# Two products of the identity with itself ahead of each pair of attention score matmuls

## The chip, the cores and the metric

The kernel runs on one core of one Trainium2 chip. The metric is the device time of one execution in microseconds (us). The kernel before was timed three times: 931.81 us (median), 927.07 us and 935.1 us.

## The reference, cut to what matters

Three stages follow one another: attention with a causal band, a gated feed-forward layer, and four experts that are all applied and weighted.

```python
# attention: q, k, v are (2, 8, 768, 64), n_global 8, n_local 96
scores = scale * np.matmul(q, k.transpose(0, 1, 3, 2))
keep = is_global | is_local            # first 8 keys, or the 96 keys up to the query
scores = np.where(keep, scores + bias, -1e9)       # bias: -slope(head) * distance
a = np.exp(scores - max); a = a / (a.sum + 1e-9)
x = np.matmul(a, v)                    # laid out as (1536, 512)
# feed-forward: w_in (512, 2048), w_out (2048, 512)
h = x @ w_in;  g = h * np.tanh(softplus(h));  x = g @ w_out
# four experts: w1 (4, 512, 1024), w2 (4, 1024, 512), p the normalised shares
out = sum(p[:, e:e + 1] * (np.maximum(x @ w1[e], 0) @ w2[e]) for e in range(4))
```

## The kernel before, in words

It is written engine by engine, with an instruction order laid down by hand and semaphores between the engines. PE is TensorE, DVE VectorE, ACT ScalarE, POOL GpSimd, SP SyncE.

**Attention** takes the 16 heads in 8 pairs of heads (m = 0 to 7). Per pair there are 12 units (u = 0 to 11): six tiles of 128 queries, and for each the two heads, so that units u and u + 1 (u even) are the two heads of one query tile. Since n_local is at most 129 and n_global at most 32, only a band of the keys is worked on: 128 keys for the first query tile, 256 for the second, 288 for the other four (the tile before, the own tile and 32 global keys). A unit goes through these steps:

- **scores** (`scores_of_two`, L517 to L524, matmul at L522): the fp32 product of q and k of both heads of a query tile. Head 0 lies in the rows 0 to 63 of the array, head 1 in the rows 64 to 127. A unit's result goes to PSUM bank u % 3. Before the matmuls, `score_parts` (L490) waits until DVE has read the unit that held the bank before (semaphore `s_ready`).
- **bias and minimum** (`biased`, DVE, L1016), **exp** (`expo`, ACT, L786), **transposes** of the 1 to 3 blocks of 128 keys (`turn`, PE, L538, fp32), the copy out as an fp16 high part (ACT, L810) and low part (DVE, L1131), and the product with v (`pv`, PE, L557, three fp16 matmuls per block).

PE's own order in a pair (`pair`, L561 to L585) is for every u: turn(u); if u is odd, the scores of the two units u + 3 and u + 4 (they reach into the next pair of heads for u = 9 and u = 11); pv of unit u - 1; and after u = 0, 2, 4, 6 a `fill` (L479), which transposes a part of q or k of the next pair. In the last pair `turn_x` (L487) stands in the places of the fills: it transposes the attention's result for the first product. `first` (L526) issues the scores of the units 0 to 3 of the first pair ahead of all. So the scores of an even unit 2, 4, 6, 8 or 10 and its neighbour are issued 40 times in all (1 from `first`, 8 x 4 at u = 1, 3, 5, 7, and 7 at u = 11), and those of unit 0 are issued 8 times.

**Beside attention** the weights are prepared. DVE takes the largest absolute value of w_in and w_out piece by piece (`weights_part`, L970: w_in beside pair 1, w_out beside pair 3). SP spreads each maximum over the partitions with two small DMAs (`share_max`, L407 to L413), behind the loads of q and k in SP's order; DVE makes a scale of it (L1068, L957 to L960; for w_out that is at u = 6 of pair 5), and POOL splits the matrix into fp16 parts with it (L707 to L713). ACT issues the load of w_out at u = 0 of pair 2 (`load_w_out`, L826).

**The rest** (from L587) is the fp16 split products of the feed-forward layer (L597, L620) and of the experts, with their elementwise work on ACT, DVE and POOL. It starts when the last attention output has been scaled (L1056).

Of the kernel before, what the change touches and what calls it, by code (L numbers as in the profile page):

```python
# [13 lines left out]
P = 128  # L14
# [22 lines left out]
def program(nc, q, k, v, n_global, n_local, w_in, w_out, probs, w1, w2, out):  # L37
    B, H, S, D = q.shape
    DM, FF = w_in.shape
    E, _, FE = w1.shape  # L40
# [18 lines left out]
    def offsets(blocks):  # L59
        at, found = 0, []  # L60
        for _, n in blocks:
            found.append(at)
            at += n
        return found, at
# [8 lines left out]
    with ExitStack() as ctx:  # L73
        def sb(name, cols, dt=F32):
            return ctx.enter_context(nc.sbuf_tensor(name, [P, cols], dt))
# [16 lines left out]
        ident = sb("ident", P)  # L92
# [11 lines left out]
        def psum(i, n=GN, at=0):  # L104

            c = 512 * (i % 2) + at
            return bank[i // 2][:, c:c + n]
# [359 lines left out]
        def _(pe):  # L467
# [22 lines left out]
            def score_parts(i, slot, u, banded):  # L490

                blks = (band if banded else full)[u // 2]
                qt, a = u // 2, u % 2
                if u == 0:

                    pe.wait_ge(tr_out, FILLS * (2 * i + slot + 1))
                if banded and (u >= 3 or not isinstance(i, int) or i + slot > 0):
                    pe.wait_ge(s_ready, PB * i + UNITS * slot + u - 2)
                offs, _ = offsets(blks)

                runs = []
                for (kt, n), at in zip(blks, offs):
                    if runs and runs[-1][0] + runs[-1][1] == kt * P and n == P and (at % 512 or not at):
                        runs[-1][1] += P
                    else:
                        runs.append([kt * P, n, at])
                head = slice(a * D, (a + 1) * D)
                return [(psum(u % 3, n, at) if banded else bank[0][:, at:at + n],
                         qT_sb[slot][head, qt * P:(qt + 1) * P], kT_sb[slot][head, key:key + n])
                        for key, n, at in runs]  # L510
# [6 lines left out]
            def scores_of_two(i, slot, u):  # L517

                parts = [score_parts(i, slot, u + a, True) for a in range(2)]
                for n in range(len(parts[0])):  # L520
                    for a in range(2):
                        last = pe.matmul(*parts[a][n], start=True, stop=True)  # L522
                        if n == len(parts[0]) - 1:
                            last.then_inc(s_psum, 1)  # L524

            def first(banded):  # L526
                if banded:
                    scores_of_two(0, 0, 0)
                    scores_of_two(0, 0, 2)
# [31 lines left out]
            def pair(i, slot, banded):  # L561
                for u in range(UNITS):
                    if not banded:
                        scores(i, slot, u, banded)
                    turn(i, slot, u, banded)
                    if banded:
                        ahead, behind = reach(i, slot, u, 3), reach(i, slot, u, -1)
                        if ahead and u % 2:
                            scores_of_two(*ahead)
                        if behind:  # L570
                            pv(*behind, banded)
                    else:
                        pv(i, slot, u, banded)
                    if after(i, slot) and u in FILL_AT:
                        fill(*after(i, slot), FILL_AT.index(u))
                    if not after(i, slot) and u in X0_TURN_AT:
                        c = X0_TURN_AT.index(u)
                        if c == 0:
                            pe.wait_ge(o_ready, 2 + 2 * (PAIRS // 2))
                            pe.wait_ge(tr_out, FILLS * PAIRS)  # L580
                        else:
                            pe.wait_ge(x_ready, c)
                        turn_x(0, c)
                if banded and not after(i, slot):
                    pv(i, slot, UNITS - 1, banded)  # L585
# [781 lines left out]
```

## Time and profile before

| | |
|---|---|
| runs | 931.81 us median (927.07 to 935.1) |
| the profiled execution's own time | 928.6 us |
| its span | 926.8 us |
| mean granted TensorE clock | 0.985 of full speed |
| PE busy | 877.1 us (95% of the span) |
| DVE busy | 524.3 us (57%) |
| ACT busy | 301.4 us (33%) |
| POOL busy | 266.4 us (29%) |
| attention, by PE's timeline | 11 us to 168.6 us |

The span goes from the first to the last instruction; the execution's own time has 1.8 us around it. A granted clock of 1.0 is 2.4 GHz, one of 0.5 is 1.2 GHz. Matmuls are pipelined, and a row's duration of one includes its way through the array, so that several in a row take less than their durations together.

### The profile page before, as it was taken

How to read it: one execution, taken by the hardware profiler on the slowest of the kernel's cores; microseconds unless marked ns; L12 is line 12 of the kernel's file. 1: busy time of each engine (PE TensorE's matmuls, PEld its weight loads, DVE VectorE, ACT ScalarE, POOL GpSimd, SP SyncE). 2: the span in 40 equal slices, each digit the busy share in tenths (PEclk: the TensorE clock that was granted, in tenths of full speed). 3: DMA queues.
4: the chain of work that ended last, by engine and by line, in shares of the span. 5: the costliest groups of instructions: out<-in, count | busy, mean ns of one | idle time of the engine just before them, and what ended most of it. 6: DMA issues, size and time to landing. Idle time of an engine off the chain costs nothing.

```text
span 926.8 us, 12448 instructions
## 1 busy us (share of the span) xinstructions
PE 877.1 (95%) x4880; PEld 441.9 (48%) x4880; DVE 524.3 (57%) x1032; ACT 301.4 (33%) x559; POOL 266.4 (29%) x218
## 2 busy tenths in 40 slices
PE   4887887899999999999999999999999999999998
PEld 3665666544444444444444444444444444444443
DVE  7888866799999999997643214322125322212121
ACT  3565766554455556555020201011010201111020
POOL 1267758022222232231007700049100094000000
PEclk9898989999999999999999999999999999999999
DMA  9735250000000000020100130000400000000001
GB/s 222 233 89 170 66 186 1 1 1 1 1 0 6 4 1 1 4 91 25 70 6 1 57 124 1 6 0 0 181 1 1 6 0 0 0 23 23 34 12 47
DMA packets 52579, 39.30 MB, mean 42 GB/s; under 512 B 41136, under 2 KB 42288, under 8 KB 52016
## 3 DMA queue, kind: packets, MB, share of 16 engines
q1 hardware_dynamic: 50464, 34.44, 12.6%
q10 hardware_dynamic: 2064, 4.19, 1.3%
q8 instruction: 30, 0.49, 0.2%
q14 instruction: 21, 0.17, 0.1%
HBM read 35.48 MB, written 3.15 MB: 42 GB/s over the span
## 4 chain that ended last, share of the span: by engine, by line
PE 66%; DVE 23%; ACT 4%; DMA 4%; issue 2%; POOL 0%; SPq 0%; DVEq 0%; ACTq 0%
PE bank L597 57%; PE bank L620 4%; DVE tmp L1244 4%; DVE tmp L1262 2%; DVE wpieces L970 2%; DVE xT L1260 2%; DVE tmp L1242 2%; DMA wB<-in_moe_w_out 2%; DVE tmp L1248 2%; PE bank L522 2%; PE bank L557 1%; PE bank L538 1%; DVE hid L1254 1%; DVE tmp L1131 1%; ACT tmp L892 1%
## 5 line engine op out<-in xcount | busy, mean ns | idle before, releaser
L597 PE MATMUL bank<-xT,wA 128*128 128x512 f16 (+1 forms) x864 | 194.5, 379 | 1.1 <-DVE acc L1056 1.1
L866 ACT ACTIVATE hid<-bank 128x512 f16<-128x512 f32 x96 | 57.3, 597 | 410.8 <-PE bank L597 410.8
L1235 DVE SCALAR_TENSOR_TENSOR hid<-bank,hid 128x512 f16<-128x512 f32 x96 | 66.4, 691 | 172.5 <-ACT hid L866 172.5
L620 PE MATMUL bank<-hid,wB 128*128 128x512 f16 x576 | 132.1, 379 | 4.3 <-ACT acc L850 2.6
L597 PEld LDWEIGHTS bank<-xT,wA 128*128 128x128 f16 x864 | 84.5, 98 | 102.4 <-DVE acc L1056 1.2
L752 POOL TENSOR_TENSOR tmp<-tmp 128x512 f32<-128x512 f32 x48 | 70.2, 1462 | 196.7 <-DVE tmp L1262 196.7
L597 PE MATMUL bank<-wA,hid 128*128 128x512 f16 x576 | 125.3, 379 | 0.0
L597 PE MATMUL bank<-xT,wB 128*128 x576 | 125.3, 379 | 0.0
L597 PE MATMUL bank<-wB,hid 128*128 128x512 f16 x576 | 125.3, 379 | 0.0
L707 POOL TENSOR_SCALAR stage<-stage,sc 128x1024 f32<-128x1024 f32 x32 | 36.0, 1125 | 251.6 <-DVEq L1228 241.0
L1311 DVE SCALAR_TENSOR_TENSOR acc<-bank,pg,acc 128x512 f32<-128x512 f32 x36 | 27.0, 750 | 131.7 <-PE bank L597 131.7
L620 PEld LDWEIGHTS bank<-hid,wB 128*128 128x128 f16 x576 | 56.1, 98 | 73.0 <-DVE hid L1254 3.5
L597 PEld LDWEIGHTS bank<-xT,wB 128*128 128x128 f16 x576 | 56.4, 98 | 67.9
L597 PEld LDWEIGHTS bank<-wA,hid 128*128 128x128 f16 x576 | 56.4, 98 | 68.0
L597 PEld LDWEIGHTS bank<-wB,hid 128*128 128x128 f16 x576 | 56.3, 98 | 68.0
L886 ACT ACTIVATE hid<-tmp 128x512 f16<-128x512 f32 x48 | 30.3, 630 | 106.5 <-POOL tmp L752 104.6
L597 PE MATMUL bank<-xT,hid 128*128 (+1 forms) x288 | 63.3, 379 | 0.0
L786 ACT ACTIVATE tmp<-tmp 128x288 f32<-128x288 f32 (+2 forms) x96 | 48.5, 505 | 36.2 <-DVE tmp L1016 34.9
L1131 DVE SCALAR_TENSOR_TENSOR tmp<-bank,tmp 128x384 f16<-128x384 f32 (+2 forms) x96 | 46.9, 489 | 23.2 <-ACT tmp L810 23.0
L557 PE MATMUL bank<-xT,tmp 128*128 128x65 f16 x720 | 41.4, 202 | 15.4 <-DVE tmp L1131 14.7
L522 PE MATMUL bank<-hid 64*128 64x256 f32 (+2 forms) x320 | 42.2, 377 | 10.9 <-DVE tmp L1016 10.3
L1244 DVE SCALAR_TENSOR_TENSOR tmp<-tmp 128x512 f32<-128x512 f32 x48 | 48.3, 1007 | 1.6
(105 smaller groups left out, 939.1 us busy)
## 6 DMA issues: line engine op xcount, KB each, us to landing
stage<-in_moe_w SPq DMA_DIRECT2D x8, 2048.0 KB, 10.1
stage<-in_moe_w_in SPq DMA_DIRECT2D x1, 4096.0 KB, 14.3
wB<-in_moe_w_out ACTq DMA_DIRECT2D x1, 4096.0 KB, 18.4
hid<-in_q SPq DMA_DIRECT2D x16, 192.0 KB, 3.5
hid<-in_k SPq DMA_DIRECT2D x16, 192.0 KB, 3.4
xT<-in_v SPq DMA_DIRECT2D x8, 384.0 KB, 4.9
out_y<-acc SPq DMA_DIRECT2D x12, 256.0 KB, 2.0
rows<-max SPq DMA_DIRECT2D x4, 128.0 KB, 4.1
```

The lines of the kernel that those rows point to most:

```text
L522: last = pe.matmul(*parts[a][n], start=True, stop=True)
L557: last = pe.matmul(dst, pt[:, x, b * P:(b + 1) * P], v_parts(m)[:, y, a, kt], start=(b == 0 and n == 0), stop=(b == len(keys) - 1 and n == 2))
L597: last = pe.matmul(dst, lhs(c, a), rhs(c, b), start=(c == 0 and n == 0), stop=(c == chunks - 1 and n == 2))
L620: last = pe.matmul(psum(4 + d), w_out_s[:, a, f // 2, f % 2, d * P:(d + 1) * P], hv[:, T % RING, b, :], start=(f == 0 and n == 0), stop=(f ...
L707: pool.tensor_scalar(tmp, src, scale, 1.0, ALU.mult, ALU.mult).then_inc(w_part, 1)
L752: pool.tensor_tensor(g_t[T % 4], g_t[T % 4], r_t[T % 2], ALU.mult).then_inc(g_ready, 1)
L786: act.activation(t, t, ACT.Exp, bias=nmax[:, u:u + 1], scale=-1.0).then_inc(p_ready, 1)
L866: act.activation(hv[:, f, 0, :], psum(f % 4), ACT.Relu).then_inc(f_hi, 1)
L886: act.activation(hv[:, m % RING, 0, :], g_t[m % 4], ACT.Copy).then_inc(h_hi, 1)
L1131: dve.scalar_tensor_tensor(pt[:, 1], src, P_SCALE, pt[:, 0], ALU.mult, ALU.subtract).then_inc(pT_dve, 1)
L1235: dve.scalar_tensor_tensor(hv[:, f, 1, :], psum(f % 4), 0.0, hv[:, f, 0, :], ALU.max, ALU.subtract).then_inc(f_ready, 1)
L1244: dve.scalar_tensor_tensor(n, u, 2.0, u, ALU.add, ALU.mult).then_inc(n_ready, 1)
```

## The change

In `scores_of_two`, which is called with the first of the two units, u, PE multiplies the fp32 identity (128 x 128) by itself twice before the score matmuls, where u is not 0. The product goes to the first 128 columns of PSUM bank u % 3. The scores of unit u are written to the same place afterwards and start afresh there, so the product is never read. It stands behind the waits of `score_parts` for both units.

```diff
@@ -517,6 +517,8 @@
             def scores_of_two(i, slot, u):
 
                 parts = [score_parts(i, slot, u + a, True) for a in range(2)]
+                for _ in range(2 if u else 0):
+                    pe.matmul(psum(u % 3, P), ident[:], ident[:], start=True, stop=True)
                 for n in range(len(parts[0])):
                     for a in range(2):
                         last = pe.matmul(*parts[a][n], start=True, stop=True)
```

## Rows read from the trace of the kernel before

**Rows 1.** The page, part 2: granted TensorE clock in 40 slices, in tenths.

```profile
PEclk9898989999999999999999999999999999999999
```

**Rows 2.** Busy time in four stretches: stretch, length, then each engine (instructions), granted clock, DMA share, GB/s.

```profile
48.00:52.00 4.00, 3.03 (x37) 2.46 (x37) 4.00 (x9) 2.39 (x7) 3.61 (x7) 1.00 0.02 4
...
104.00:108.00 4.00, 3.84 (x51) 3.27 (x50) 2.53 (x10) 3.60 (x9) 3.83 (x4) 1.00 0.00 0
...
128.00:132.00 4.00, 4.00 (x37) 2.96 (x35) 2.55 (x9) 1.61 (x5) 3.73 (x4) 0.50 1.04 388
...
200.00:220.00 20.00, 20.00 (x94) 9.02 (x93) 19.14 (x28) 8.99 (x15) 5.30 (x4) 1.00 0.00 0
```

**Rows 3.** The chain that ended last, in order of time: start, us, what.

```profile
61.78 18.38 DMA wB<-in_moe_w_out
...
105.34 0.77 PE bank L522 x8
...
117.28 6.04 DMA rows<-max
```

**Rows 4.** Groups of instructions up to 220 us: busy, mean ns; idle before.

```profile
L522 PE MATMUL bank<-hid 64*128 64x256 f32 x160 | 32.3, 483 | 7.4 <-DVE tmp L1016 7.3
```

**Rows 5.** Line L538 by itself: duration in ns, min/median/max, first and last start in us.

```profile
L538 PE MATMUL bank<-ident,tmp x240: 272/273/477, 15.5 to 165.3; 128*128 128x128 f32 x120
```

**Rows 6.** PE's instructions in order of time: start, us, what; scores and transposes.

```profile
98.07 0.70 PE L522 MATMUL bank<-hid 64*128 64x256 f32 x4
...
108.70 0.53 PE L538 MATMUL bank<-ident,tmp 128*128 128x128 f32 x3
...
109.79 0.49 PE L522 MATMUL bank<-hid 64*128 64x128 f32 x4
...
127.03 0.80 PE L522 MATMUL bank<-hid 64*128 64x128 f32 x4
...
130.25 1.23 PE L522 MATMUL bank<-hid 64*128 64x256 f32 x4
```

**Rows 7.** The same view: the starts of attention and of pair 1.

```profile
19.86 1.49 PE L522 MATMUL bank<-hid 64*128 64x256 f32 x8 [2.86 <-DVE tmp L1016]
...
38.67 1.22 PE L522 MATMUL bank<-hid 64*128 64x256 f32 x4 [0.40 <-DVE tmp L1016]
```

**Rows 8.** The same view: PE's waits ahead of slow stretches, and one ahead of none.

```profile
82.17 0.32 PE L557 MATMUL bank<-xT,tmp 128*128 128x65 f16 x3 [3.15 <-DVE tmp L1131]
...
125.75 0.65 PE L557 MATMUL bank<-xT,tmp 128*128 128x65 f16 x9 [2.48 <-DVE tmp L1131]
...
152.36 0.98 PE L487 MATMUL bank<-ident,acc 128*128 128x128 f32 x4 [1.85 <-DVE xT L1116]
...
158.17 0.66 PE L487 MATMUL bank<-ident,acc 128*128 128x128 f32 x4 [1.50 <-DVE xT L1116]
```

**Rows 9.** DVE's instructions in order of time: its two waits for DMAs.

```profile
80.19 1.22 DVE L970 TENSOR_REDUCE wpieces<-wB 128x1 f32<-128x1024 f32 x1 [2.95 <-DMA wB<-in_moe_w_out]
...
123.34 0.29 DVE L1068 TENSOR_REDUCE sc<-rows 128x1 f32<-128x128 f32 x1 [1.31 <-DMA rows<-max]
```

**Rows 10.** PE in order of time: pair 4 from pv(7) to the fill; pair 5's fill; a wait there.

```profile
109.06 0.44 PE L557 MATMUL bank<-xT,tmp 128*128 128x65 f16 x9
...
113.75 0.63 PE L479 MATMUL bank<-ident,hid 128*128 128x128 f32 x4
...
118.41 0.66 PE L479 MATMUL bank<-ident,hid 128*128 128x128 f32 x4 [0.16 <-ACT hid L776]
...
132.38 0.63 PE L479 MATMUL bank<-ident,hid 128*128 128x128 f32 x4
```

**Rows 11.** PE in order of time: two like stretches of the last pair.

```profile
156.24 0.44 PE L557 MATMUL bank<-xT,tmp 128*128 128x65 f16 x9
...
160.51 0.44 PE L557 MATMUL bank<-xT,tmp 128*128 128x65 f16 x9
```

## The prediction

> **What bounds the kernel now.** I read the clock of the page first, then busy time by stretches, then the chain of waits, then PE's and DVE's instructions in order of time. The change touches attention alone, so the question is what attention (11 to 168.6 us) waits for. The clock dips only there: in the first 7 of 40 slices [rows 1]. After it PE is busy all the time at the full clock, as in 200:220 [rows 2], and nothing catches up, so a microsecond lost or won in attention is one of the total. Within attention the bound changes. In most pairs it is PE: 3.84 of 4 us busy, DVE 2.53 (104:108); where DVE reduces weights (pairs 1 and 3) it is DVE: 4.00 of 4, PE 3.03 (48:52) [rows 2]. The score matmuls themselves stand in the chain, at 105.34 [rows 3]. Two DMAs stand there as well: the load of w_out, 18.38 us, and the spread of its maximum [rows 3]; at their ends DVE has waited 2.95 and 1.31 us [rows 9]. In front of these a delay of PE can vanish.
>
> **Price of one visit** (two identity products). A fp32 matmul is two instructions: 160 records for the 80 matmuls of 256 columns [rows 4]. Four instructions of 128 columns take 0.49 us, four of 256 take 0.70 us [rows 6]. The heads run side by side in two halves of the rows, so 0.21 us is what 128 more columns cost in two instructions: 0.105 us each. The identity fills all rows, nothing runs beside it: two products are four instructions, 4 x 0.105 = 0.42 us. That is the lower end; I exclude less, as PE takes them in order. Transposes of the same shape follow each other at (0.53 - 0.273) / 2 = 0.13 us [rows 5, 6], which would make 0.51. I take **0.50**, nearer the transposes since they too fill the array. The upper end is a weight load that hides behind nothing: after its own 0.21 us of columns, the 0.49 us group has 0.28 us left for one load and the way through the array; bounding the load by 0.11 us, as long as the columns, gives 8 x 0.107 = 0.86. At half clock the same difference is 1.23 - 0.80 = 0.43 [rows 6], so a visit costs 0.86 to 1.0 there; I take 0.90.
>
> The overlap of weight load and matmul is where a rule speaks against the change. The trace has full-array transposes 0.13 us apart, hardly above their columns. The Trainium skill (TensorE: Matmul & The Clock Gate, Part 3, "The mechanism") says that weight loads overlap running matmuls only where the row groups differ; the identity fills them all, so by that rule the sum would be that of 0.86.
>
> **The visits, in order.** There are 40, so 80 products.
> - Hidden, 17. One from `first`: DVE then works on v, and PE idles 2.86 us before 19.86 [rows 7]. Pair 0 at u = 5 and 7, pair 1 at 3, 5 and 7, pair 3 at 3, 5 and 7: DVE-bound, in 48:52 PE has 4.00 - 3.03 = 0.97 us to spare [rows 2] and scores are issued three units ahead. All of pair 2 (5) and pair 3 at u = 1: DVE waits 2.95 us for w_out at their end [rows 9]. Four of them lie plainly on PE's path, 2.0 us; were they dearer than 0.74 each, this cover would be gone and the surplus counted. Pair 5 at u = 7: issued before the wait for the scale of w_out. The last pair at u = 3: PE idles 1.85 us soon after, until 152.36, for DVE [rows 8].
> - At half clock, 4. Pair 0 at u = 1 and 3: the scores take 1.49 us there [rows 7], though the page's clock shows nothing low so early. 2 x 0.90 = 1.8, but the rise of the clock comes at the same moment, and the 1.8 us of work pushed behind it takes half: 0.9. The visits at 38.67 (pair 0, u = 11) and after it (pair 1, u = 1): 1.8, less the same effect for part of it and DVE's own reductions: 1.0. Sum 1.9.
> - On PE's path at full clock, 19. Pair 1 and pair 3 at u = 11 (2), pair 4 (5), pair 5 at u = 1, 3, 5 (3) and u = 11 (1), pair 6 (5), the last pair at u = 1, 5, 7 (3): 19 x 0.50 = 9.5. Five of these (pair 4 from u = 7 on, to pair 5 at u = 5) lie between SP's issue of the last q and k and the end of the DMA that spreads w_out's maximum; this runs by itself and DVE waits 1.31 us for it [rows 9], so 1.3 comes off. The short waits for ACT's copies ahead of fills (0.16 us, once in each of some 4 pairs) [rows 10] come off: 0.6.
>
> Sum: 1.9 + 9.5 - 1.3 - 0.6 = **9.5 us**. SP's loads of q and k shift with PE, but their buffers are double. POOL's split of w_out shifts with DVE's scale; it ends near 161 us and is needed four steps into the rest, near 185: hidden. DVE and ACT wait for later scores and do nothing extra.
>
> **What the clock gives back.** PE falls to half clock after waits of 3.15, 2.48 and 1.85 us, and not after 1.50 [rows 8]. With the change, PE is later by about 2.5 at the first of these while the DMA is not, which leaves some 0.7; at the second 1.3 + 0.5 go, leaving 0.7. I expect both falls to vanish. At the first DVE bounds: 0.3. At the second PE does: from pv(7) to the fill it takes 132.38 - 125.75 = 6.63 us at 0.50 [rows 2, 8, 10] and 113.75 - 109.06 = 4.69 in pair 4 [rows 10]: 1.9. Net: 9.5 - 0.3 - 1.9 = **+7.3 us**. The other falls have no visit in the wait before them and stay.
>
> **Rivals.**
> 1. **All of attention at full clock.** The added work is dense and might lift every low stretch. Then also: last pair, (156.24 - 152.36) - (160.51 - 158.17) = 1.5 [rows 8, 11]; an estimate for the three stretches around 20, 40 and 57 us: scores take 1.22 against 0.70 [rows 6, 7], and the transposes and pv between them as much again, so 1.0 to 1.1 each, 3.2 together; and the cold visits cost about 1 less. 7.3 - 5.7 = **+1.6 us**, 933.4. Against: the waits before these falls hold no visit. For: PE ran at full clock through all of pair 4, where it was busiest [rows 2]. The Trainium skill (same page, Part 1, "What's actually happening") says the same in general: "the default state is throttled, and activity releases the throttle"; by it two products per visit could only help, most where PE has the longest waits. Chance 0.17.
> 2. **Slower: weight loads don't hide.** Place: between the four identity instructions. Visit 0.86: cold 3.0, 19 x 0.86 = 16.3, less 1.3 and 0.6, plus 0.9 where pair 2 outgrows its cover, less 2.2 by the clock: **+16 us**, 948. It passes 1% once a visit costs 0.60. For: the rule above. Against: the spacing of transposes. Chance 0.18.
> 3. **The clock doesn't react**: all falls stay, **+9.5 us**, 941.3, on the border. Chance 0.15.
> 4. **Two products are swallowed** (the compiler drops what is never read, or PE has more air than I count): 0 to 3 us, 933. The waits say PE has none in most pairs. Chance 0.08.
>
> **How the numbers follow.** The forecast, +7.3, has 0.42. The profiled execution took 928.6 us, so its like would be 935.9; it stands 3.2 below the median of the runs, which I take as the base: 931.8 + 7.3 = **939.1 us**. Within the forecast the price, 0.42 to 0.56, moves it by 2 to 3 us. The range reaches from rivals 1 and 4 (933) to short of rival 2, **932.5 to 947**. A measurement of this kernel tells about 1% (9.3 us) from no change. Faster by over 1% only if rival 1 is far richer than its rows: 0.03. Slower by over 1%: rival 2, half of rival 3 and some of the forecast, 0.18 + 0.08 + 0.08 = 0.34. Within: 0.63.
>
> **What the new profile would show.** 160 more records of 128*128 128x128 f32 at the new line. Scores of pair 4 spaced by 0.50 more than before; a group of identity instructions of 0.42 to 0.56 us ahead of them (rival 2: 0.8 or more). DVE's wait for w_out shrinks from 2.95 to about 1 and its wait for the maximum from 1.31 to 0. PE's wait near 126 us falls under 1 us and the half clock behind it is gone; the last attention output ends 7 us later. I am wrong in the clock if low stretches stay behind short waits, or go where no visit is near, and wrong in the cover if pair 2's delay shows at the w_out wait.

## The result, and the profile after

The changed kernel takes 935.61 us (median of 20 runs, 933.19 to 938.11); the kernel before, run as often, 931.25 us (927.07 to 935.1). The ratio is 1.0054, 95% interval 1.004 to 1.0068: 5.0 us slower (3.7 to 6.3). That lies in the forecast range, has the forecast sign, and is inside the 1% that was called no change. The forecast, +7.3, lies above the interval.

The granted clock in 40 slices (page, part 2) answers to [rows 1]: of three dips in the first six slices, two are left.

```profile
PEclk9898999999999999999999999999999999999999
```

Next, the products by themselves (duration in ns min/median/max, first and last start), and the groups of PE up to 225 us (busy, mean ns; idle before), in the trace after.

```profile
L521 PE MATMUL bank<-ident x160: 275/275/582, 14.3 to 164.1; 128*128 128x128 f32 x160
...
L559 PE MATMUL bank<-xT,tmp 128*128 128x65 f16 x720 | 39.2, 197 | 7.6 <-DVE tmp L1133 7.0
...
L524 PE MATMUL bank<-hid 64*128 64x256 f32 x160 | 30.5, 460 | 0.0
L521 PE MATMUL bank<-ident 128*128 128x128 f32 x160 | 28.6, 306 | 7.9 <-DVE tmp L1018 7.8
```

The same group of pv in the kernel before:

```profile
L557 PE MATMUL bank<-xT,tmp 128*128 128x65 f16 x720 | 41.4, 202 | 15.4 <-DVE tmp L1131 14.7
```

All 160 instructions run; nothing was dropped. The wait that stood before the scores (7.4 us in [rows 4]) stands before the products now. PE's idle time before pv has halved, from 15.4 to 7.6 us: part of what the products take was idle time. Each instruction of a product has a weight load of its own, 192 ns long (median), where the transposes' take 141 ns:

```profile
L540 PEld LDWEIGHTS bank<-ident,tmp x240: 137/141/231, 16.6 to 170.4; 128*128 128x128 f32 x120
L521 PEld LDWEIGHTS bank<-ident x160: 186/192/337, 14.3 to 164.0; 128*128 128x128 f32 x160
```

PE after, in order of time (start, us, what; idle before), at the places of [rows 6 to 8], with pair 4's scores at u = 9 and the start of the rest:

```profile
38.99 1.19 PE L521 MATMUL bank<-ident 128*128 128x128 f32 x4 [0.60 <-DVE tmp L1018]
...
79.07 1.19 PE L521 MATMUL bank<-ident 128*128 128x128 f32 x4 [2.49 <-DVE tmp L1018]
...
102.52 0.70 PE L524 MATMUL bank<-hid 64*128 64x256 f32 x4
...
104.44 0.61 PE L521 MATMUL bank<-ident 128*128 128x128 f32 x4
104.98 0.84 PE L524 MATMUL bank<-hid 64*128 64x256 f32 x8
...
115.30 0.49 PE L524 MATMUL bank<-hid 64*128 64x128 f32 x4
...
131.28 0.43 PE L559 MATMUL bank<-xT,tmp 128*128 128x65 f16 x9 [0.87 <-DVE tmp L1133]
...
158.27 0.66 PE L487 MATMUL bank<-ident,acc 128*128 128x128 f32 x4 [1.58 <-DVE xT L1118]
...
173.89 4.45 PE L599 MATMUL bank<-xT,wA 128*128 128x512 f16 x12 [1.07 <-DVE acc L1058]
```

The products start 0.54 us before the scores that they precede (104.44 to 104.98). From the scores just before pair 4's u = 0 to those at its u = 9 took 109.79 - 98.07 = 11.72 us [rows 6] and now takes 115.30 - 102.52 = 12.78: 1.06 us for the four visits between, 0.27 each. The wait near 126 us is 0.87 instead of 2.48 us [rows 8], as forecast (under 1 us).

DVE after, where it needs the results of three DMAs (the two of [rows 9], and one more, for the scale of w_in), and the load of w_out in the chain:

```profile
76.97 0.29 DVE L1070 TENSOR_REDUCE sc<-rows 128x1 f32<-128x128 f32 x1 [1.33 <-DMA rows<-max]
...
84.08 1.22 DVE L972 TENSOR_REDUCE wpieces<-wB 128x1 f32<-128x1024 f32 x1 [1.15 <-DMA wB<-in_moe_w_out]
...
128.86 0.29 DVE L1070 TENSOR_REDUCE sc<-rows 128x1 f32<-128x128 f32 x1
```

```profile
62.75 21.30 DMA wB<-in_moe_w_out
```

The granted clock, as one column before the last two (stretches of 4 us):

```profile
80.00:84.00 4.00, 4.00 (x32) 3.10 (x31) 1.05 (x4) 0.76 (x4) 3.83 (x4) 0.50 1.02 288
...
128.00:132.00 4.00, 3.13 (x41) 2.55 (x38) 2.92 (x13) 2.27 (x7) 1.85 (x2) 1.00 1.01 409
...
172.00:176.00 4.00, 2.55 (x15) 1.19 (x16) 1.37 (x6) 0.00 (x0) 0.00 (x0) 0.76 0.01 4
```

128:132 has the full clock where [rows 2] has 0.50. 80:84 is still at half, behind the 2.49 us wait at 79.07. And 172:176 is new: the first matmuls of the rest run low in this execution. Attention ends 173.89 - 168.62 = 5.27 us later by PE's first matmul of the rest (168.62 in the trace before); the span grew by 934.0 - 926.8 = 7.2, the other 1.9 lying behind that point. Most of it is that low clock: the first twelve matmuls of the rest take 4.45 us (the last line of PE's rows above), and 2.76 in the trace before:

```profile
168.62 2.76 PE L597 MATMUL bank<-xT,wA 128*128 128x512 f16 x12 [1.07 <-DVE acc L1056]
```

How the 5.27 us come about shows in the start of the scores for unit 0 of the next pair, which are issued at u = 9 of each pair (the last line is the start of the rest):

| at u = 9 of | before, us | after, us | later by, us |
|---|---|---|---|
| pair 0 | 34.56 | 34.88 | 0.32 |
| pair 1 | 56.99 | 58.57 | 1.58 |
| pair 2 | 71.91 | 74.17 | 2.26 |
| pair 3 | 95.81 | 99.70 | 3.89 |
| pair 4 | 109.79 | 115.30 | 5.51 |
| pair 5 | 127.03 | 132.00 | 4.97 |
| pair 6 | 142.49 | 147.59 | 5.10 |
| the rest | 168.62 | 173.89 | 5.27 |

Pair 3 takes on the shift of the w_out load and nothing more: the load lands 3.89 us later (DVE's first reduction of it at 80.19 before and 84.08 after), and the pair ends 3.89 us later. The load began 0.97 us later (61.78 to 62.75), and took 21.30 instead of 18.38 us.

### The profile page after: what moved, and what is told of

The parts are those of the page before. It is cut to its first block, busy times and chain, and to the rows that moved or that the text cites. A ratio compares the mean times of both kernels' runs of the same rounds, so it can differ in the third digit from the quotient of the medians.

```text
span 934.0 us, 12768 instructions
## 1 busy us (share of the span) xinstructions
PE 891.9 (95%) x5040; PEld 458.1 (49%) x5040; DVE 525.2 (56%) x1032; ACT 300.5 (32%) x559; POOL 266.0 (28%) x218
## 4 chain that ended last, share of the span: by engine, by line
PE 66%; DVE 23%; DMA 4%; ACT 3%; issue 2%; POOL 0%; SPq 0%; DVEq 0%; ACTq 0%
PE bank L599 57%; PE bank L622 4%; DVE tmp L1246 4%; DVE tmp L1264 2%; DVE xT L1262 2%; DMA wB<-in_moe_w_out 2%; DVE wpieces L972 2%; DVE tmp L1244 2%; DVE tmp L1250 2%; DVE hid L1256 1%; PE bank L524 1%; DVE tmp L1133 1%; PE bank L559 1%; PE bank L540 1%; DVE tmp L1018 1%
## 5 line engine op out<-in xcount | busy, mean ns | idle before, releaser
L812 ACT ACTIVATE tmp<-bank 128x384 f16<-128x384 f32 (+2 forms) x96 | 41.4, 432 | 27.0 <-PE bank L540 26.8
L972 DVE TENSOR_REDUCE wpieces<-stage 128x1 f32<-128x1024 f32 x40 | 47.4, 1210 | 0.0
## 6 DMA issues: line engine op xcount, KB each, us to landing
wB<-in_moe_w_out ACTq DMA_DIRECT2D x1, 4096.0 KB, 21.3
```

The lines of the kernel that those rows point to most:

```text
L812: act.activation(pt[:, 0], src, ACT.Copy, scale=P_SCALE).then_inc(pT_act, 1)
L972: dve.tensor_reduce(wpieces[:, c:c + 1], src[:, at:at + PIECE], AX_X, ALU.max, apply_absolute_value=True).then_inc(w_piece, 1)
```

## The experiments

Single executions scatter by several us, and their mean granted clock with them, so each kernel's clock is averaged over all its executions and stands beside its time. Those of the kernel before (23 executions beside the first four experiments) have clocks from 0.970 to 0.989, mean 0.981; time falls by 3.7 us per 0.01 of clock, correlation -0.70 (3.0 and 2.8 us in the 31 and 14 beside the others). The 20 of the changed kernel have 0.990. The 926.8 us profile, with 0.985 and 928.6 us, was better than the mean of its kernel.

The recorded clock has a gap of its own. In the traces of two kernels below, "all waits" and "uncovered visits only", the scores near 20 us take the 1.49 us of the low clock in both, but for 12 to 28 us the first has a granted clock of 1.00 on record and the second 0.68 (the row of "all waits" first):

```profile
19.83 1.49 PE L522 MATMUL bank<-hid 64*128 64x256 f32 x8 [2.86 <-DVE tmp L1032]
```

```profile
12.00:28.00 16.00, 10.85 (x62) 8.46 (x64) 12.84 (x38) 6.84 (x16) 0.41 (x1) 1.00 1.09 268
```

```profile
21.01 1.49 PE L524 MATMUL bank<-hid 64*128 64x256 f32 x8
```

```profile
12.00:28.00 16.00, 10.78 (x76) 8.80 (x76) 12.51 (x37) 7.18 (x16) 0.41 (x1) 0.68 1.11 267
```

That alone is 0.32 x 16 / 930 = 0.0055 of mean clock without a difference in time. So small differences of mean clock are rough, and a clock near 1 doesn't say that this first stretch ran at full speed.

The theory: a visit costs PE's time, less what short gaps absorb, and part is given back because activity in PE's waits keeps the clock up. The rivals: the clock is a bystander; or what is paid is that the scores come later than pv and the other work of their step.

| kernel | ratio to before, 95% interval | as us of 930.7 | mean clock |
|---|---|---|---|
| changed kernel | 1.0054 (1.004 to 1.0068) | +5.0 | 0.990 |
| four products | 1.0126 (1.0095 to 1.0158) | +11.7 | 0.995 |
| pairs 4 and 6 only | 1.002 (0.9997 to 1.0044) | +1.9 | 0.981 |
| behind pv | 1.0046 (1.0024 to 1.0069) | +4.3 | 0.991 |
| half the columns | 1.0078 (1.0049 to 1.0107) | +7.3 | 0.984 |
| eight waits | 0.9971 (0.9948 to 0.9993) | -2.7 | 0.994 |
| one wait | 1.0001 (0.9975 to 1.0028) | +0.1 | 0.983 |
| covered visits only | 0.9996 (0.9971 to 1.002) | -0.4 | 0.989 |
| uncovered visits only | 1.0069 (1.0041 to 1.0097) | +6.4 | 0.984 |
| all waits | 0.9949 (0.9932 to 0.9966) | -4.7 | 0.997 |
| all waits, transposes | 0.9947 (0.9927 to 0.9967) | -4.9 | 0.997 |

**Four products.**

```diff
-                for _ in range(2 if u else 0):
+                for _ in range(4 if u else 0):
```

> Four products per visit instead of two, same 40 visits. Theory (PE's work sets the cost, 0.45 us per two products at full clock, about 0.12 us of the first two vanishes in short gaps of PE): the second two have no gaps left, so 19 visits x 0.45 = 8.5 us more than the changed kernel's +5, and pair 2 outgrows the wait for w_out: about +14 us over the kernel before (12 to 17), at a granted clock no lower than 0.99. Rival (the change is cheap because activity buys clock): the rest of the low stretches goes as well, and the total stays at or below +8.

+11.7 us. PE in its trace, in pair 4:

```profile
104.93 1.06 PE L521 MATMUL bank<-ident 128*128 128x128 f32 x8
105.92 0.84 PE L524 MATMUL bank<-hid 64*128 64x256 f32 x8
```

The scores start 0.99 us after the products, 0.45 later than with two: the price of two products, near the lower end (0.42) that was set from [rows 6], not the 0.50 chosen. The total is a little under the 12 to 17 expected, and the rival's +8 or less lies outside the interval (8.8 to 14.7). Twice the activity pushed the clock only from 0.990 to 0.995; the second two products cost 6.7 us more, the first two 5.0. The stretch of pair 4 that took 11.72 us before and 12.78 with two products takes 117.33 - 103.01 = 14.32 with four: 0.27 us per visit for the first two, 0.39 for the second two, which find less left to be absorbed in.

```profile
103.01 0.70 PE L524 MATMUL bank<-hid 64*128 64x256 f32 x4
...
117.33 0.49 PE L524 MATMUL bank<-hid 64*128 64x128 f32 x4
```

**Two products, only ahead of the scores of pairs 4 and 6.**

```diff
-                for _ in range(2 if u else 0):
+                for _ in range(2 if u and 2 * i + slot in (4, 6) else 0):
```

> Two products, only ahead of the scores of pairs 4 and 6 (10 visits), where PE is the busiest engine and next to no low clock lies. Theory: 0.33 us per visit as in the changed kernel's trace (0.45 less 0.12 in gaps), and some of pair 4 disappears in the wait for the maximum of w_out: +3 us (2 to 4). Rival (a visit costs its full 0.5 and the clock gave the rest back elsewhere): +5 us.

+1.9 us, interval -0.3 to +4.1, at the clock of the kernel before. Ten visits at 0.5 would be 5 us, which the interval excludes. Read from the traces (0.27 at eight of them, and 0.56 at the two of u = 11, see the section on the prediction), they come to 3.3 us, less some cover by the wait for the maximum. That agrees, but the interval also holds 0, so it doesn't settle more.

**Behind pv.**

```diff
                         if behind:
                             pv(*behind, banded)
+                        if u % 2 and u != 9:
+                            filler(u - 1, 2)
...
+            def filler(v, n):
+                for _ in range(n):
+                    pe.matmul(psum(6 + v // (UNITS // 2), 112, 400), ident[:], ident[:, 0:112], start=True, stop=True)
```

> Two products of 112 columns behind the pv of the same step instead of ahead of the scores (39 places, into unused columns of the bank that pv has just written). Theory (PE's time is what is paid): like the changed kernel, +4 to +6 us. Rival (what is paid is the later arrival of the scores at DVE): the scores now come as early as before, and the total falls to +2 or less.

+4.3 us (2.2 to 6.4): as dear as the change within the intervals, with 112 columns instead of 128, in 40 places (160 instructions in the trace; the expectation says 39). It lies a little outside the rival's +2 or less. Where in the step the products stand makes no difference that these runs can tell: what is paid is PE's time. In both kernels all that stands behind the products in PE's order comes later.

**Half the columns.**

```diff
-                    pe.matmul(psum(u % 3, P), ident[:], ident[:], start=True, stop=True)
+                    pe.matmul(psum(u % 3, P // 2), ident[:], ident[:, 0:P // 2], start=True, stop=True)
```

> The two products have 64 columns instead of 128; the weight is still the whole identity. Theory A (columns set the price, loads hide behind them): a visit costs 0.21 to 0.25 us and the total falls to about +1 to +2 us. Theory B (four loads of 128 columns of fp32 weights follow each other at about 0.1 us each, as long as the columns): a visit stays at 0.4 us or more and the total at +4 to +5. A group of four instructions would show 0.55 us or more under B, about 0.4 under A (0.61 in the changed kernel).

```profile
105.38 0.56 PE L521 MATMUL bank<-ident 128*128 128x64 f32 x4
105.87 0.84 PE L524 MATMUL bank<-hid 64*128 64x256 f32 x8
```

0.49 us instead of 0.54 for half of the columns: the columns don't set this price. The weight loads are the same as before, 192 ns each (median):

```profile
L521 PEld LDWEIGHTS bank<-ident x160: 186/192/338, 14.3 to 164.0; 128*128 128x128 f32 x160
```

This is what theory B says; another fixed time per fp32 instruction would look the same and wasn't tested apart. The total, +7.3 us (4.6 to 10.0), misses both expectations upwards. The clock is 0.984 instead of 0.990 in all six executions: PE is held for nearly as long and, it seems, less clock is bought. The intervals of this kernel and the changed one overlap, so the extra 2 us are not shown.

**Eight waits.** No visit has products; 48 products of 112 columns stand in PE's long waits (`filler` as above).

```diff
                         if ahead and u % 2:
+                            filler(u - 2, {(0, 9): 5, (1, 9): 3}.get((m, u), 0))
                             scores_of_two(*ahead)
                         if behind:
+                            filler(u - 1, {(0, 10): 4, (1, 10): 3, (3, 2): 12, (5, 8): 9}.get((m, u), 0))
                             pv(*behind, banded)
...
+                                filler(u - 1, {(7, 4): 7, (7, 8): 5}.get((m, u), 0))
                             pe.wait_ge(x_ready, c)
```

> No product ahead of any score. Instead products of 112 columns run only where the trace of the kernel before shows PE waiting longest (48 in 8 places: pair 0 at u = 9 and 10, pair 1 at u = 9 and 10, pair 3 at u = 2, pair 5 at u = 8, the last pair at u = 4 and 8), sized to fit into the wait. Theory (a visit costs PE's time, and activity in the waits buys clock at about 3.5 us per 0.01 of granted clock, as the runs of the kernel before scatter): nothing is paid, the mean clock rises from 0.981 to 0.990 or more and the time falls by 3 us or more. Rival (the clock is a bystander, the scatter has another cause): the time stays within 1 us of the kernel before, whatever the clock does.

-2.7 us (-4.8 to -0.7), clock 0.994: faster than the kernel before, with more work. The clock is no bystander. In its profile the rest still began low:

```profile
166.90 5.30 PE L607 MATMUL bank<-xT,wA 128*128 128x512 f16 x12 [1.07 <-DVE acc L1066]
```

**One wait** keeps only the entry (5, 8): 9.

> Only one of those places: 9 products of 112 columns at u = 8 of pair 5, in the 2.48 us wait ahead of 125.75 us. Theory: the low stretch behind it goes, about 1.9 us where it occurs; since other low stretches stay, -1 to -2 us and the clock up by about 0.005. Rival: 0.

+0.1 us (-2.3 to +2.6), clock 0.983: not resolved, and the clock rose by 0.002, not by the 0.005 expected. Its profile has the full clock behind the filled wait and half clock later, near 153 us, as the kernel before:

```profile
128.00:132.00 4.00, 3.63 (x53) 2.60 (x54) 3.81 (x16) 3.21 (x9) 3.73 (x4) 1.00 1.03 394
...
152.00:156.00 4.00, 3.40 (x36) 2.90 (x34) 1.56 (x7) 2.31 (x5) 3.73 (x4) 0.65 0.02 4
```

One low stretch is worth about 2 us by the prediction's rows, may not occur in every execution, and the others stay: twelve executions can't tell that from 0.

**Covered visits only, and uncovered visits only.** Two products ahead of the scores only where this condition on pair and unit holds (the first kernel, 16 visits), or only where it doesn't (the second, 23 visits). The one of `first` has none in either.

```diff
-                for _ in range(2 if u else 0):
+                for _ in range(2 if (2 * i + slot, u) in {(0, 8), (0, 10), (1, 6), (1, 8), (1, 10), (2, 4), (2, 6), (2, 8), (2, 10), (3, 2), (3, 4), (3, 6), (3, 8), (3, 10), (5, 10), (7, 6)} else 0):
```

> Two products only at the 16 visits inside attention that the prediction called hidden. If the cover holds: 0 us or, with some clock bought, -1 to -2. If it doesn't: up to 16 x 0.33 = 5 us slower.

-0.4 us (-2.7 to +1.9), clock 0.989: no net cost, and 5 us are excluded. But the clock rose by 0.008 as well, worth about 2 us by the prices below, so the covered visits may have cost something that this gave back.

> Two products only at the 23 visits that the prediction put on PE's path. Theory: these carry the whole cost; as less clock is bought than by all 40, +5 to +7 us, at least what the changed kernel costs (+5). Rival (the cost is spread over all visits): +3 us.

+6.4 us (3.8 to 9.1), clock 0.984, as expected and more than the rival's +3: the 23 visits that were put on PE's path carry the cost. That it is more than the change's 5.0, because the covered visits buy clock, fits but isn't shown: the intervals overlap. The two kernels together make +6.0.

**All waits**, the eight and 14 more places (the expectation counts 13), 95 products in all; the last two of them:

```diff
+                    filler(UNITS - 1, 2)
                     pv(i, slot, UNITS - 1, banded)
+                    for _ in range(4):
+                        pe.matmul(psum(0, 112), ident[:], ident[:, 0:112], start=True, stop=True)
```

> The eight filled waits, and 13 more places: the DVE-bound steps of pairs 1 and 3, the scores ahead of pair 3, three more waits of the last pair, and 4 products of 112 columns in the wait between attention and the rest, where the first twelve matmuls of the rest took 5.3 us instead of 2.8 in some profiles. Theory (activity in PE's waits buys clock and costs nothing): clock 0.996 or more, -5 us against the kernel before (-4 to -7). Rival (what could be bought is bought already, and new products now delay PE): no better than the eight places, -3 us, or worse.

-4.7 us (-6.3 to -3.2), clock 0.997. The page of that trace, part 2, and the start of the rest:

```profile
PEclk9999999999999999999999999999999999999999
```

```profile
164.83 1.12 PE L601 MATMUL bank<-ident 128*128 128x112 f32 x8
166.07 2.76 PE L613 MATMUL bank<-xT,wA 128*128 128x512 f16 x12
```

The first twelve matmuls of the rest take 2.76 us, where they took 5.30 with eight waits filled. That the products just ahead did it is not shown: the trace of the kernel before has 2.76 too, without any.

**All waits, transposes.**

```diff
-                for _ in range(n):
-                    pe.matmul(psum(...), ident[:], ident[:, 0:112], start=True, stop=True)
+                for _ in range(n + (n + 1) // 2):
+                    pe.transpose(psum(...), ident[0:112, :], ident[0:112, 0:112])
```

> The same places filled for the same time with fp32 transposes of the identity (3 for 2 products) instead of products. If any activity of PE counts for the clock: like the kernel with products, -5 us. If transposes don't count (the Trainium skill says so in TensorE: Matmul & The Clock Gate, Part 4, of its own kernels): clock near 0.981, 0 us.

The last place has 6 transposes instead of 4 products. -4.9 us (-6.8 to -3.1), clock 0.997, median 925.89 us: level with the kernel with products. Its profile has one instruction per transpose; the rest still waits 0.47 us for DVE behind the last of them:

```profile
L564 PE MATMUL bank<-ident 112*128 112x112 f32 x143 | 17.9, 265 | 0.0
```

```profile
165.74 2.76 PE L613 MATMUL bank<-xT,wA 128*128 128x512 f16 x12 [0.47 <-DVE acc L1072]
```

## Why the prediction was right

Direction and place were right: PE's time in attention, partly covered, partly given back by the clock. The size came out within the range although the price on PE's path was set too high, and one of its single waits came true by luck. By its steps:

- **Cover: held, as far as the rows show it.** DVE-bound pair 1: pv's waits before and after,

```profile
47.55 0.34 PE L557 MATMUL bank<-xT,tmp 128*128 128x65 f16 x6 [1.14 <-DVE tmp L1131]
...
55.42 0.43 PE L557 MATMUL bank<-xT,tmp 128*128 128x65 f16 x9 [0.85 <-DVE tmp L1131]
```

```profile
49.13 0.34 PE L559 MATMUL bank<-xT,tmp 128*128 128x65 f16 x6 [0.66 <-DVE tmp L1133]
...
57.00 0.43 PE L559 MATMUL bank<-xT,tmp 128*128 128x65 f16 x9 [0.24 <-DVE tmp L1133]
```

  are 1.58 us later at both points: the two visits between are free, and come out of the waits. The three in pair 3 behind the landing of w_out are free as well: it lands 3.89 us later, and the pair ends 3.89 later. Pair 2 did show some of its visits, 1.58 to 2.26 us, ahead of DVE's wait for w_out, which took them in. The covered visits by themselves cost -0.4 us net, with the reserve said there.
- **Half-clock visits: 1.9 forecast**, and these same 1.58 us are what attention had lost by then, the covered visits of pairs 0 and 1 included.
- **The price, and with it the term of the 19 visits (19 x 0.50 = 9.5 us): mis-sized.** The scores start 0.45 us later for two more products, not 0.50; and of that pair 4 shows 1.06 / 4 = 0.27 per visit. "PE has none in most pairs" was wrong: there is slack that the waits don't show. PE's idle time in that stretch fell from 11.72 - 11.41 = 0.31 to 12.78 - 12.72 = 0.06 us:

```profile
98.07:109.79 11.72, 11.41 (x145) 9.25 (x144) 8.76 (x35) 9.84 (x25) 11.30 (x8) 1.00 0.12 27
```

```profile
102.52:115.30 12.78, 12.72 (x161) 11.22 (x160) 8.45 (x32) 9.14 (x24) 10.79 (x8) 1.00 0.14 33
```

  and more was hidden in what counts as busy, since a row's duration runs on while nothing new starts. The pv behind a lone transpose started 0.43 us after it before, and 0.14 after:

```profile
98.99 0.30 PE L538 MATMUL bank<-ident,tmp 128*128 128x128 f32 x1
99.42 0.43 PE L557 MATMUL bank<-xT,tmp 128*128 128x65 f16 x9
```

```profile
103.45 0.30 PE L540 MATMUL bank<-ident,tmp 128*128 128x128 f32 x1
103.59 0.44 PE L559 MATMUL bank<-xT,tmp 128*128 128x65 f16 x9
```

  Not every visit finds such slack. Those at u = 11 cost more than the forecast price: from the scores at u = 9 of pair 3 to those at u = 11 it was 98.07 - 95.81 = 2.26 us and is 102.52 - 99.70 = 2.82, 0.56 more, and pairs 4 and 6 show 0.57 and 0.56. So the 19 visits come to 14 x 0.27 + 5 x 0.56 = 6.6 us, an estimate from these rows, where 9.5 less 0.6 for short waits were forecast. Rival 2, weight loads that don't hide, is out: a load takes 0.19 us, four of them 0.77, and the scores follow four instructions at 0.54 and eight at 0.99 us.
- **DMA waits.** w_out: 2.95 to 1.15 us, "about 1", but by luck. The forecast had PE 2.5 us later there and the DMA not. In fact DVE came to this wait 5.7 us later (82.93 instead of 77.24), and the load landed 3.9 us later. The maximum: 1.31 to 0, as forecast. But a third wait appeared, 1.33 us for w_in's scale, which the sum didn't have. In the traces of the experiments it comes and goes without regard to the edit: 1.07 in pairs 4 and 6 only and none with one wait, whose code is the old one up to there. The w_out load's length does so too: 18.4 us before, and 19.1 to 21.3 in all the others, 21.2 with pairs 4 and 6 only and 20.0 with one wait. So both belong to the scatter, and the trace before had the shortest load of all, which is probably a part of why the two traces are 7.2 us apart and the kernels 5.0.
- **Clock.** The fall near 126 us went with its wait, as forecast: from pv(7) to the fill it took 6.63 us and now takes 136.15 - 131.28 = 4.87, with the products of one visit in it.

```profile
136.15 0.63 PE L479 MATMUL bank<-ident,hid 128*128 128x128 f32 x4
```

  The fall near 80 was to vanish; in the profile it only moved to the other side of a new wait. The ones near 57 and 153 were to stay, and are gone, the second behind a wait of 1.58 us; and a low start of the rest is there that wasn't. With pairs 4 and 6 only, the stretch near 57 has the full clock too, with the old code up to there. So which stretch is low can't be forecast from one execution. Over many, the mean clock rose from 0.981 to 0.990. What 0.01 of clock is worth comes from the two kernels that only fill waits, if their products cost nothing: 2.7 / 1.3 = 2.1 and 4.7 / 1.6 = 2.9 us. The 0.009 bought are then some 1.9 to 2.6 us, where 2.2 were forecast. That is an estimate, as the intervals of these times are wide and the recorded clock is rough. Gross cost by it: 5.0 + 2.3 = 7.3 instead of 9.5; by the visits, 1.6 + 6.6 - 1.3 = 6.9.

Rival 1, all at full clock for +1.6 us, didn't occur by this change; even four products, at a clock of 0.995, cost 11.7 us. What it rests on is real: with products in the waits and none in the way, the clock reached 0.997, and the time fell below the kernel before. Rival 3, a clock that doesn't react, is out by the same runs, and its +9.5 us lies outside the interval. Of rival 4, nothing was dropped, but its "more air than I count" is what made the price too high.

## What to carry to other kernels

Work that is added only to keep a clock up belongs into the waits of the engine, not ahead of its critical instructions: 80 products at the visits gave +5 us, 95 of much the same kind in the waits -5 us. Read the mean clock of many executions before costing such an edit, since a single profile shows a draw. And small additions can cost less than their instruction time even where a stretch looks 96% busy: 0.27 us for 0.45 at four visits out of five, though 0.56 at the fifth. The spacing of the starts shows it, the busy share doesn't.

## What the runs showed of the hardware

- fp32 transposes in the waits bought as much clock (0.997 instead of 0.981) as fp32 products, and as much time (-4.9 and -4.7 us). The Trainium skill (TensorE: Matmul & The Clock Gate, Part 4) says of its own kernels that transposes don't count; here the measurement decides, and they do.
- Two full-array fp32 products of 64 columns hold up what follows for hardly less time than two of 128 (0.49 and 0.54 us); their weight loads are equally long, 192 ns each. Those of fp32 transposes of the same size take 141 ns.
- The clock can be low at the head of a dense stretch of matmuls: 5.30 against 2.76 us for the same twelve. Both occur behind the same wait of 1.07 us (eight waits, and the kernel before); what decides between them stays open.
- The granted clock on record can be 1.00 where the durations are those of the low clock: 1.49 us for the scores near 20 us, with 1.00 on record in one trace and 0.68 over 12 to 28 us in another.
